# Routed expert layers on one core: record fetches from Pool, raw weight loads at ring pace, split rate by tile count

## The reference

```python
def _moe2_ref(x, w_gate, w_output_gate, w1, w2):      # x: 4608 x 512, w1: 8 x 512 x 1024, w2: 8 x 1024 x 512
    logits = x @ w_gate
    e_idx = np.argmax(logits, axis=1)
    ...                                               # gate_w: softmax weight of e_idx, eom: sigmoid(x @ w_output_gate)
    for e in range(E):
        mask = e_idx == e
        h = np.maximum(x[mask] @ w1[e], 0.0)
        out[mask] = gate_w[mask, None] * eom[mask, e, None] * (h @ w2[e])
```

## Time and profile before

| what | us |
|---|---|
| time, median of 3 executions | 1148.81 |
| lowest and highest of the three | 1148.08 and 6159.94 |
| the profiled execution's own time | 1147.24 |
| its span, from first to last instruction | 1145.5 |

### The profile page before, as it was taken

How to read it: one execution, slowest core, us unless ns; L and a number is a source line. 1 busy time by engine, 2 the same in 40 slices (tenths; PEclk the granted TensorE clock), 3 DMA queues, 4 the chain that set the end, 5 groups by cost and what they waited for, 6 DMA issues and landing times.

```text
span 1145.5 us, 22549 instructions
## 1 busy us (share of the span) xinstructions
PE 1080.0 (94%) x6180; PEld 896.5 (78%) x6181; DVE 585.1 (51%) x1217; ACT 382.1 (33%) x644; POOL 216.4 (19%) x375
## 2 busy tenths in 40 slices
PE   4899999999999999999992999999999999999695
PEld 3688888888888888888882888888888888888584
DVE  6866767666675767666654333424333332332420
ACT  3433334333333334333330333324333332342321
POOL 2443211202120211202122011111111111111110
PEclk9899999999999999999996999999999999999898
DMA  7541232212221132212001444332423242142000
GB/s 225 183 139 59 62 74 73 63 47 74 73 62 62 60 73 73 64 46 74 29 19 47 120 131 128 126 119 80 124 92 125 77 136 84 54 137 75 28 30 28
DMA packets 57270, 96.70 MB, mean 84 GB/s; under 512 B 15759, under 2 KB 15887, under 8 KB 57233
## 3 DMA queue, kind: packets, MB, share of 16 engines
q1 hardware_dynamic: 47168, 75.60, 21.7%
q0 software_dynamic: 7968, 20.61, 6.1%
q10 hardware_dynamic: 2096, 0.04, 0.1%
HBM read 76.66 MB, written 20.60 MB: 85 GB/s over the span
## 4 chain that ended last, share of the span: by engine, by line
PE 91%; DVE 2%; DMA 2%; issue 1%; ACT 1%; SPq 0%; POOL 0%; ACTq 0%; DVEq 0%; POOLq 0%
PE Y_ps L431 37%; PE H_ps L431 36%; PE T L423 6%; PE S_ps L480 3%; PE X_ps L490 3%; PE L_ps L458 3%; PE X_ps L423 2%; PE S_ps L423 2%; DMA stage<-in_k 1%; ACT x L623 1%; DVE wx L684 1%; DMA stage<-in_moe_w_out 0%; DMA prob<-x_rows,slot_rec 0%; DVE dl L684 0%; POOL route_table L1010 0%
## 5 line engine op out<-in xcount | busy, mean ns | idle before, releaser
L431 PE MATMUL Y_ps<-wx,dh 128*128 (+1 forms) x1216 | 386.3, 399 | 2.7 <-DVE dl L684 2.6
L431 PE MATMUL H_ps<-wx,xh 128*128 (+1 forms) x1216 | 336.5, 399 | 12.2 <-DVE wx L684 8.7
L431 PEld LDWEIGHTS H_ps<-wx,xh 128*128 128x128 f32 x1216 | 225.0, 190 | 57.6 <-issue 11.8
L431 PEld LDWEIGHTS Y_ps<-wx,dh 128*128 128x128 f32 x1216 | 220.1, 188 | 49.5 <-issue 8.1
L431 PE MATMUL Y_ps<-wx,dl 128*128 (+1 forms) x608 | 238.2, 392 | 0.0
L431 PE MATMUL H_ps<-wx,xl 128*128 (+1 forms) x608 | 188.7, 392 | 0.0
L684 DVE TENSOR_TENSOR wx<-stage,wx (+1 forms) x63 | 76.6, 1225 | 156.9 <-ACT wx L637 156.3
L431 PEld LDWEIGHTS H_ps<-wx,xl 128*128 128x128 f32 x608 | 115.0, 189 | 25.1
L431 PEld LDWEIGHTS Y_ps<-wx,dl 128*128 128x128 f32 x608 | 114.1, 188 | 25.4
L564 ACT ACTIVATE stage<-T 64x512 f32<-64x512 f32 x36 | 21.3, 592 | 206.7 <-PE T L423 167.4
L716 DVE TENSOR_REDUCE nmax_h<-H_ps 128x1 f32<-128x1024 f32 x36 | 44.1, 1224 | 86.1 <-PE H_ps L431 86.1
(11 more groups left out here) (161 smaller groups left out, 1252.7 us busy)
## 6 DMA issues: line engine op xcount, KB each, us to landing
stage<-in_moe_w SPq DMA_DIRECT2D x128, 256.0 KB, 3.0
stage<-in_q SPq DMA_DIRECT2D x36, 256.0 KB, 2.9
stage<-in_k SPq DMA_DIRECT2D x72, 128.0 KB, 3.1
stage<-in_v SPq DMA_DIRECT2D x36, 256.0 KB, 3.2
x_rows<-x SPq DMA_DIRECT2D x36, 256.0 KB, 2.0
stage<-in_moe_w_out SPq DMA_DIRECT2D x4, 512.0 KB, 3.9
stage<-in_moe_w_in SPq DMA_DIRECT2D x3, 512.0 KB, 8.5
slot_rec<-route_table SPq DMA_DIRECT2D x40, 2.0 KB, 1.6
```

The costliest lines, as they stand in the source:

```text
L431: i = pe.matmul(acc[:, c0:c0 + HALF], x[:, kk, :], w(part, kk * cols + c0), start=first and x is hi and part == 0, stop=last and x is lo)
```

## The change

Three edits in the third stage. SP's fetches of slot records move to POOL, behind the scatter in each slot. i_load becomes the same as i_split, less eight at the end of the list: SP requests raw piece p+8 as soon as p is split, for all pieces that the slot is due to split, with no other bound. And the constant rate of two pieces a slot becomes a rate for each expert by its number of tiles: 2 for four tiles or more, 3 for three, 4 for two, 8 for one. With `pace` = rate x (idx + 1) - 2, mid is min(pace, 8), or 0 in an expert's first slot, and the end is min(pace + 1, 8).

```diff
--- before.py
+++ after.py
@@ -25,8 +25,6 @@
 PIECES = 8
 PW = WC // PIECES
 RING = 8
-SPLIT_RATE = 2
-LOAD_RATE = 2
 
 
 def at_least(eng, sem, count):
@@ -371,14 +369,6 @@
 
             steps(sp.Fori, step)
 
-            sp.wait_ge(bases_set, 1)
-            sp.wait_ge(rec_st, 16 * NT)
-
-            def load_rec(c, u):
-                s = c * 4 + u
-                base = sp.value_load(i_base[0:1, bass.ds(s, 1)], min_val=0, max_val=TROWS - P)
-                sp.dma_start(slot_rec[u % 4][:, :], table[bass.ds(base, P), :]).then_inc(rec_in[u % 4], 16)
-
             def load_raw(p):
 
                 e = sp.value_load(i_act[0:1, bass.ds(p // PIECES, 1)], min_val=0, max_val=NE - 1)
@@ -392,11 +382,6 @@
 
             def slot(c, u, has):
                 s = c * 4 + u
-                if has(3):
-                    if has(-1):
-
-                        sp.wait_ge(out_st[(u + 3) % 4], uses(c, u - 1, 4) * 16)
-                    load_rec(c, u + 3)
                 if has(0) or isinstance(s, int) and s == -1:
                     lo = bound(sp, i_load, s, RING) if has(0) else 0
                     hi = bound(sp, i_load, s + 1, RING)
@@ -407,8 +392,6 @@
                             wait_alone(sp, raw_in, (p + RING) * 32, passed)
                             load_raw(p + RING)
 
-            for s in range(2):
-                load_rec(0, s)
             sp.wait_ge(slots_set, 1)
             sp.sem_inc(raw_in, PIECES * 32)
             slot_steps(sp, slot)
@@ -847,9 +830,10 @@
             link, n = linker(slot_chain, 0)
             dve.wait_ge(rt_rec, NCH)
             tiles, ends, gap, act1, rank, zero = (temp(NE) for _ in range(6))
+            rate, rate1 = temp(NE), temp(NE)
             past, wide1, below = (temp(SLOTS * NE).rearrange("o (j e) -> o j e", e=NE) for _ in range(3))
-            n_past, base, idx, kk, mid, own = (temp(SLOTS) for _ in range(6))
-            till, first, least = (temp(SLOTS + 1) for _ in range(3))
+            n_past, base, idx, kk, mid, own, pace = (temp(SLOTS) for _ in range(7))
+            till = temp(SLOTS + 1)
             limit, limit8 = temp(1), temp(1)
             acts, ranks = temp(NE * NE).rearrange("o (r e) -> o r e", e=NE), temp(NE)
 
@@ -889,9 +873,19 @@
             dve.tensor_scalar(i_act[:, :], ranks, float(NE - 1), None, ALU.min)
 
 
-            link(dve.tensor_scalar(idx, idx, float(SPLIT_RATE), None, ALU.mult))
-            dve.tensor_scalar(mid, idx, float(PIECES), float(PIECES), ALU.min, ALU.add)
-            link(dve.tensor_scalar(idx, idx, 1.0, float(PIECES), ALU.add, ALU.min))
+            dve.tensor_scalar(rate, tiles, 3.5, 2.0, ALU.is_lt, ALU.add)
+            link(dve.tensor_scalar(rate1, tiles, 1.5, 4.0, ALU.is_lt, ALU.mult))
+            link(dve.scalar_tensor_tensor(rate, tiles, 2.5, rate, ALU.is_lt, ALU.add))
+            link(dve.tensor_tensor(rate, rate, rate1, ALU.add))
+            link(dve.tensor_tensor(rate1[:, 0:NE - 1], rate[:, 1:], rate[:, 0:NE - 1], ALU.subtract))
+            link(dve.tensor_tensor(wide1[:, :, 0:NE - 1], past[:, :, 0:NE - 1], rate1[:, 0:NE - 1].unsqueeze(1).to_broadcast([1, SLOTS, NE - 1]), ALU.mult))
+            link(dve.tensor_reduce(pace, wide1[:, :, 0:NE - 1], AX.X, ALU.add))
+            link(dve.tensor_scalar(pace, pace, rate[:, 0:1], None, ALU.add))
+            link(dve.scalar_tensor_tensor(pace, idx, 1.0, pace, ALU.add, ALU.mult))
+            link(dve.tensor_scalar(pace, pace, -2.0, None, ALU.add))
+            link(dve.scalar_tensor_tensor(mid, idx, 0.5, pace, ALU.is_gt, ALU.mult))
+            dve.tensor_scalar(mid, mid, float(PIECES), float(PIECES), ALU.min, ALU.add)
+            link(dve.tensor_scalar(idx, pace, 1.0, float(PIECES), ALU.add, ALU.min))
             dve.scalar_tensor_tensor(mid, kk, float(PIECES), mid, ALU.mult, ALU.add)
             link(dve.tensor_scalar(own, kk, float(PIECES), float(PIECES), ALU.mult, ALU.add))
             link(dve.tensor_tensor(till[:, 1:], own, idx, ALU.add))
@@ -901,14 +895,8 @@
             link(dve.tensor_tensor(till[:, 1:SLOTS], till[:, 1:SLOTS], own[:, 1:], ALU.max))
             link(dve.tensor_copy(till[:, 0:1], own[:, 0:1]))
 
-            dve.tensor_scalar(first[:, 0:SLOTS], s_j[:, :, 0], 2.0, float(LOAD_RATE), ALU.add, ALU.mult)
-            dve.memset(first[:, SLOTS:], float((SLOTS + 2) * LOAD_RATE))
-            dve.tensor_scalar(least[:, SLOTS:], till[:, SLOTS:], float(-PIECES), None, ALU.add)
-            link(dve.tensor_scalar(least[:, 0:SLOTS], mid, float(-PIECES), None, ALU.add))
-            link(dve.tensor_tensor(least, least, first, ALU.max))
-            link(dve.tensor_tensor(least, least, till, ALU.min))
             dve.tensor_copy(i_split[:, :], till)
-            dve.tensor_scalar(i_load[:, :], least, limit8, None, ALU.min).then_inc(slots_set, 1)
+            dve.tensor_scalar(i_load[:, :], till, limit8, None, ALU.min).then_inc(slots_set, 1)
 
 
             def low(src, hi, lo):
@@ -1017,6 +1005,11 @@
             pool.wait_ge(st_x2[0], 16 * NT // 2)
             pool.wait_ge(st_x2[1], 16 * NT // 2)
 
+            def load_rec(c, u):
+
+                base = pool.value_load(i_base[0:1, bass.ds(c * 4 + u, 1)], min_val=0, max_val=TROWS - P)
+                pool.dma_start(slot_rec[u % 4][:, :], table[bass.ds(base, P), :]).then_inc(rec_in[u % 4], 16)
+
             def gather(c, u):
 
                 wait_alone(pool, rec_in[u % 4], uses(c, u, 4) * 16, passed)
@@ -1033,6 +1026,14 @@
                     wait_alone(pool, y_ev, s, passed)
                     pool.indirect_dma_start(out, bass.IndirectOffsetOnAxis(ap=slot_rec[(u + 3) % 4][:, 1:2].bitcast(u32), axis=0),
                                             yb[(u + 1) % 2][:, :], None, bounds_check=TOK - 1, oob_is_err=False).then_inc(out_st[(u + 3) % 4], 16)
+                if has(3):
+                    if has(-1):
+                        wait_alone(pool, out_st[(u + 3) % 4], uses(c, u - 1, 4) * 16, passed)
+                    load_rec(c, u + 3)
+            pool.wait_ge(bases_set, 1)
+            pool.wait_ge(rec_st, 16 * NT)
+            for i in range(2):
+                load_rec(0, i)
             gather(0, 0)
             last = slot_steps(pool, slot)
             for b in range(4):
```

## The result

The changed kernel takes 1141.27 us (median of 5 executions, 1140.77 to 1142.27), against 1148.08 us for the kernel before over five (1148.81 over the three shown). The ratio is 0.9941, with a 95% interval of 0.9927 to 0.9954: 6.8 us less.

What follows compares the result with a forecast made beforehand. PE was taken as the bound, busy 94% of the span. Span 1145.5 - 4.0 (stall) + 0.7 (start) = 1142.2 us, plus 1.74 to time and 1.57 to median, gave 1145.5 us, range 1142.5 to 1150.

Steps and rivals of the forecast that it cites:

- The stall: PE's wait for split weights before slot 36's first product, behind a six-piece burst: from 8.7 to 4.1 us.
- The new wait for dl: Slot 34's product with w2 waits for DVE's dl, pushed back by two more low parts: 0.55 us.
- The burst steps of 0.95 and 1.13 us: In a burst of split pieces, ACT starts one every 0.95 us and DVE one every 1.13 us.
- The start: Before the first product, POOL's first record fetch delays slot 0's gather: 0.7 us cost, between -0.5 and +4.1.
- the longer table: Thirteen added operations delay slots_set by some 1.8 us, covered by the gather of slot 0, so nothing is paid.
- Record fetches on POOL: Moving fetches from SP to POOL costs 0.7 us at the start and zero in the steady slots.
- The clock: Granted clock still falls in the shorter stall; the next product's 1.93 us loss stays, so 0 gained (ends 0 to 1.93).
- The rival in which the clock holds: Clock stays up or recovers sooner after the shorter stall: up to 1.93 us more gained, about 1143.6 us; chance 0.12.
- Raw pieces at ring pace: Earlier raw-piece requests gain nothing and may meet a gather in flight: zero, within 0.5 us either way.
- The start cost: Rival: POOL's first fetch lands late and delays slot 0's gather, +5.1 us, so 1149.9 us; chance 0.15.
- become the chain: Rival: POOL's scatter, fetch and gather outlast each slot's slack, 0.7 us in about 36 slots: 1171 us; chance 0.04.
- Nothing comes of it: Rival: PE's wait moves to DVE's dl and relu in slots 34 and 35: 1148.8 to 1149.5 us; chance 0.10.

Runs made afterwards that it cites:

- c_only: Kernel before with only the split rate by tile count (table of slots longer, SP still fetching records): 1144.80 us, ratio 0.9960.
- a_only: Kernel before with only the record fetches moved from SP to POOL, old table of slots: 1145.62 us, ratio 0.9968.
- one_per_slot: Kernel before, records still fetched by SP, plus one spare plain POOL DMA in each slot, 40 in all: 1143.64 us, ratio 0.9955.
- first_by_sp: Changed kernel with the first three record fetches given back to SP, the other 37 on POOL: 1140.03 us, ratio 0.9929 to the kernel before.
- b_only: Kernel before with only the raw-piece loads by ring place, the old bound on requests lifted: 1163.14 us, ratio 1.0138.
- four_four_b: Repeat: changed kernel, first three fetches by SP, rate 5 instead of 4 for two tiles: 1138.56 us, ratio 0.9907 to the kernel before.
- four_four: Changed kernel, first three fetches by SP, rate 5 instead of 4 for two tiles: 1139.66 us, ratio 0.9911 to the kernel before.
- slots_18: Kernel before with 18 spare plain POOL DMAs of 2 KB among slots 0 to 3: 1150.54 us, ratio 1.0015.
- first_by_sp_b: Repeat of the changed kernel with the first three record fetches given back to SP: 1140.21 us, ratio 0.9924 to the kernel before.

## Why the prediction was wrong

**What it had right.** The bound and its place. The stall: the wait was forecast to go from 8.7 to 4.1 us, and went to 4.2, and to 4.1 in c_only. The new wait for dl: 0.55 us forecast, 0.64 measured. The net gain between the end of the first product and H_ps of slot 36: 4.0 us forecast, 3.7 in the ledger. The burst steps of 0.95 and 1.13 us carried over. The start: 0.7 us forecast, 0.67 measured from the last scatter of records to the first product, partly by luck. The forecast took the longer table as covered, and c_only shows that it alone delays the gather by 0.6 us; the two delays don't add. (The table's own delay was forecast as 1.8 us and is 1.7 behind the last scatter, though three old operations go beside the group for `least`, and not one.) The fetch itself landed in 2.07 us where SP's took 1.63. By the page "DMA: Bandwidth & Descriptors" of the Trainium skill (section "Specifications") it was to be 0.4 us more. That this difference agrees says little: with the old table POOL's took 1.85 us (a_only) against 1.59 to 1.83 for SP's, and with the longer one SP's took 1.86 to 2.22.

**The step that failed** is in the sum, in the words "Span 1145.5 - 4.0 + 0.7 = 1142.2 us": only the stall and the start were changed in the span, and what follows the last scatter inside it was carried over unchanged, without a word on why. (The 1.74 us between span and time lie outside it and became 1.57.) Between the issue of the last scatter and the end of the span lie 9.7 us of the kernel before, of which the scatter's landing takes 2.8. The 6.607 us of POOL's DRAIN were in the trace, in the rows of one source line, but neither the chain of waits nor the profile's page shows them as work of an engine. "Record fetches on POOL" was priced with what POOL's DMAs cost while the slots run, and not with what they leave behind. a_only and one_per_slot show the price in their place: -5.07 us. With it the sum would have been 1145.5 - 5.1 = 1140.4 us, 0.9 from the measured time. That it comes so near is luck. The span would have been 1137.1 us, and it is 1139.7: the clock took 1.9 us, the start 0.4 and Y_ps of slot 34 with its wait 0.3 more than forecast. Against that, 1.57 us were added for the median above the profiled execution, from a median of three with the 6159.94 us among them; over five executions it is 0.84 us for the kernel before, and in the changed kernel the profiled execution is itself the median.

**The clock.** I had the clock's cost unchanged. In the ledger the first product took 8.31 us instead of 7.19 (+1.12), and H_ps of slot 36 8.13 instead of 7.39 (+0.74), 1.9 us lost. But this term belongs to no edit that the runs could show: the first product took 7.10 in a_only, 7.77 in first_by_sp, 8.60 in b_only, and H_ps of slot 36 7.33 and 8.15 in two executions of the same first_by_sp kernel. It is scatter of 1 to 1.5 us on each restart after such an idle, and I gave it no width. The rival in which the clock holds did not come true; four_four_b shows that it can with less idle, and four_four that it need not.

**Raw pieces at ring pace** was right for the change and wrong as reasoned. The changed kernel shows no wait from it, but not because the bound did nothing. b_only lost 1.4% by it. The forecast had asked what earlier requests collide with on the DMA engines, and the answer was on SP's own queue. That three fetches "are off SP's list" was in the text, as a matter of half a microsecond.

**The rivals.** The start cost less than 1 us, not 5. POOL did not become the chain: PE waited for no gather behind the first. "Nothing comes of it" needed a wait for dl of 4 us, and it was 0.64. The change lies within 2%, which had 0.96.

**What stays open** is the rule by which DMAs drop out of the count n. Shown: a step of 0.0817 us; drains that fit n = 80, 81, 84, 98, 104, 71, 18 and 15; that kind and register make no difference, and that one in each slot, with POOL's waits between them, does.

## What to carry to other kernels

Follow the end of the kernel past its last product and its last DMA, to the last row of every engine: a closing DRAIN is time like any other, and an edit that adds DMAs to POOL's queue can change it by more than the stall it aims at. When a bound on prefetching is lifted, ask what else waits in the issuing engine's queue behind the transfers that it held back, and move that first. And when a burst ahead of a product is to be spread, work out the queues of both engines step by step from the rows: that part of a forecast can be right to a few tenths of a microsecond.

## What the runs showed of the hardware

- POOL's closing DRAIN grew by about 0.08 us for each DMA more that POOL issued in the slots, from 6.607 us with 80 to 8.562 us with 104, and repeated within 0.003 us between kernels with the same DMAs in the same slots. Forty more DMAs, one in each slot, made it 5.07 us shorter; forty bunched in four slots only 0.74 us.
- The clock held after 1.80 us of PE idle in one execution and fell to 0.50 in another of the same kernel on another chip, with the same wait at the same place. The first product behind 4.1 us of idle or more took 6.7 to 8.6 us, where 5.46 or 5.47 is its time at full clock.
- The fetch of slot 0's records took 1.59 to 1.83 us to land from SP with the old table of slots (eleven kernels, 1.67 or less in nine; 1.75 in one_per_slot and 1.83 in slots_18), and 1.86 to 2.22 us from SP with the longer table (c_only, first_by_sp, first_by_sp_b, four_four and four_four_b). From POOL it took 1.85 us with the old table (a_only) and 2.07 with the longer. I have no explanation.
